# Counting the tokens above fifteen search steps: 24 matmuls of one tile each, or 3 matmuls of eight tiles each and a second matmul

## The reference

```python
cap = N // E                       # 3072 // 8 = 384
logits = x @ w_gate
order = np.argsort(-logits.flatten())
for idx in order:                  # best (token, expert) pairs first
    tok, e = (int(idx) // E, int(idx) % E)
    if assigned[tok] >= 0 or counts[e] >= cap:
        continue
    assigned[tok] = e
    counts[e] += 1
for e in range(E):
    mask = assigned == e
    out[mask] = np.maximum(x[mask] @ w1[e], 0.0) @ w2[e]
```

## Time and profile before

| | |
|---|---|
| time, median of 3 runs | 931.36 us (923.73 to 933.32) |
| profiled execution | 922.0 us, span 920.0 us |
| TensorE busy | 755.5 us, 82% of the span |
| TensorE weight loads | 563.7 us, 61% |
| VectorE busy | 464.4 us, 50% |
| ScalarE, GpSimd busy | 316.7 us, 221.6 us |
| chain that ended last | PE 63%, DVE 19%, issue 5%, DMA 4% |

### The profile page before, as it was taken

How to read it: one execution, slowest core, us unless ns; L and a number is a source line. 1 busy time by engine, 2 the same in 40 slices (tenths; PEclk the granted TensorE clock), 3 DMA queues, 4 the chain that set the end, 5 groups by cost and what they waited for, 6 DMA issues and landing times.

```text
span 920.0 us, 15204 instructions
## 1 busy us (share of the span) xinstructions
PE 755.5 (82%) x5546; PEld 563.7 (61%) x5546; DVE 464.4 (50%) x1172; ACT 316.7 (34%) x586; POOL 221.6 (24%) x281
## 2 busy tenths in 40 slices
PE   0077897998893169999999999999972999999994
PEld 0066887887783135565666565566542787777783
DVE  5989999999944737474747373632111000000010
ACT  9678787886610001111112121221210222222221
POOL 0455564645250010202020201223422000000000
PEclk9998979799896559999999999999995999999997
DMA  7293866768350303131414140641119999999970
GB/s 271 44 277 92 255 149 215 174 207 233 94 126 26 138 27 138 52 137 44 146 44 146 43 147 27 226 143 42 49 43 326 327 324 330 313 326 326 324 242 10
DMA packets 94040, 151.94 MB, mean 165 GB/s; under 512 B 21845, under 2 KB 71121, under 8 KB 93216
## 3 DMA queue, kind: packets, MB, share of 16 engines
q1 hardware_dynamic: 65728, 117.48, 38.3%
q0 software_dynamic: 11520, 24.03, 9.1%
q10 hardware_dynamic: 16736, 9.68, 3.6%
HBM read 115.92 MB, written 19.53 MB: 147 GB/s over the span
## 4 chain that ended last, share of the span: by engine, by line
PE 63%; DVE 19%; issue 5%; DMA 4%; ACT 3%; SPq 2%; POOL 1%; ACTq 1%; DVEq 0%; POOLq 0%
PE bank L867 15%; PE bank L880 14%; PE bank L996 10%; PE bank L1006 9%; PE bank L820 4%; PE bank L754 3%; DMA arena<-sorted 2%; DVE arena L1055 2%; SPq L245 2%; DVE arena L1095 2%; PE bank L904 2%; DVE arena L1070 1%; DVE arena L1142 1%; PE bank L856 1%; DVE arena L1126 1%
## 5 line engine op out<-in xcount | busy, mean ns | idle before, releaser
L867 PE MATMUL bank<-arena 128*128 128x384 f32 x384 | 140.3, 506 | 4.1 <-issue 3.4
L880 PE MATMUL bank<-arena 128*128 128x384 f32 x384 | 143.0, 503 | 0.0
L754 PE MATMUL bank<-arena 96*128 96x224 f32 (+1 forms) x384 | 92.7, 406 | 23.8 <-ACT arena L529 11.1
L996 PEld LDWEIGHTS bank<-arena 128*128 128x128 f32 x864 | 100.8, 194 | 5.5 <-issue 1.0
L996 PE MATMUL bank<-arena 128*128 128x128 f32 x864 | 101.0, 278 | 0.6 <-ACT arena L707 0.6
L754 PEld LDWEIGHTS bank<-arena 96*128 96x128 f32 x384 | 81.6, 231 | 29.7 <-issue 26.3
L1006 PE MATMUL bank<-arena 128*128 128x384 f32 x288 | 98.9, 486 | 0.0
L867 PEld LDWEIGHTS bank<-arena 128*128 128x128 f32 x384 | 68.8, 192 | 41.6 <-issue 6.0
L880 PEld LDWEIGHTS bank<-arena 128*128 128x128 f32 x384 | 67.3, 190 | 32.3
L344 POOL DMA_DIRECT2D arena<-arena x132 | 73.3, 566 | 53.8 <-DVE arena L1095 45.6
L408 POOL DMA_INDIRECT arena<-rows,arena x24 | 24.7, 1031 | 234.7 <-DVE arena L1303 229.5
(11 more groups left out here) (235 smaller groups left out, 1166.2 us busy)
## 6 DMA issues: line engine op xcount, KB each, us to landing
arena<-in_moe_w SPq DMA_DIRECT2D x52, 1536.0 KB, 7.7
arena<-arena POOLq DMA_DIRECT2D x48, 144.0 KB, 3.5
arena<-arena SPq DMA_DIRECT2D x46, 144.0 KB, 3.8
arena<-in_v SPq DMA_DIRECT2D x6, 1024.0 KB, 9.9
arena<-in_a_re SPq DMA_DIRECT2D x12, 384.0 KB, 4.2
arena<-in_a_im SPq DMA_DIRECT2D x12, 384.0 KB, 4.5
arena<-in_q SPq DMA_DIRECT2D x12, 384.0 KB, 6.7
arena<-in_k SPq DMA_DIRECT2D x12, 384.0 KB, 7.6
```

The lines of the kernel that those rows point to most:

```text
L754: mm = pe.matmul(bank[i][:, to:to + width], keys[p][0:SD, j * KW + e * P:j * KW + (e + 1) * P], queries[p][0:SD, from_:from_ + width], sta ...
L867: mm = pe.matmul(pP[f % 2][:, 0:CAP], w1_sb[p][:, kt * FF + f * P:kt * FF + (f + 1) * P], xeT[p][:, kt * CAP:(kt + 1) * CAP], start=(kt == ...
L880: mm = pe.matmul((pY, pKV)[m % 2][:, 0:DM], hT[p][:, f * CAP + t * P:f * CAP + (t + 1) * P], w2_sb[p][:, f * DM:(f + 1) * DM], start=(f == ...
L996: mm = pe.matmul(slot_hidden[f % 4][:, 0:width], w1_sb[p][:, kt * FF + f * P:kt * FF + (f + 1) * P], xeT[p][:, kt * width:(kt + 1) * width ...
```

## The change

For the 45 rounds that have other work between their steps, steps 2 to 5 of the round are replaced; the 11 others stay as they are. `count_grouped` takes eight token tiles in one matmul (`GT` = 8): 120 weight columns (8 tiles x 15 steps) against 64 columns (8 tiles x 8 experts), three matmuls instead of 24. The 120 x 64 result holds wanted blocks, where the tile of the row is the tile of the column, and unwanted ones. VectorE multiplies by a mask of the wanted ones (`own_tile`), sums over the tiles to 120 x 8, and spreads each row's sums to the 15 x 8 places of its step (`own_step`, 120 x 120). `add_groups` is one f32 matmul with weights of ones (120 x 128) on 120 columns, which gives every partition the whole 15 x 8 table. VectorE then takes the maximum over the experts, compares with 384, multiplies by the bound of the step, and the maximum of the reached bounds and the old prefix is the new prefix.

```diff
+        GT = P // (TH + 1)
+        GR = GT * TH
...
+        grouped_at = tied_tiles_at + NT * E
+
+        def handing_out(ph, d):
+            return ph >= 2 or ph == 1 and d >= 3
...
+            own = own_tile[:, :].rearrange("p (j e) -> p j e", e=E)
+            link(pool.memset(own_tile[:, :], 1.0))
+            link(pool.affine_select(out=own, in_=own, compare_op=ALU.is_ge, fill=0.0,
+                                    base=0, pattern=[[-TH, GT], [0, E]], channel_multiplier=1))
+            link(pool.affine_select(out=own, in_=own, compare_op=ALU.is_ge, fill=0.0,
+                                    base=TH - 1, pattern=[[TH, GT], [0, E]], channel_multiplier=-1))
+            link(pool.memset(own_step[:, :], 0.0))
+            for j in range(GT):
+                link(pool.affine_select(out=own_step[:, :], in_=own_step[:, :], compare_op=ALU.not_equal, fill=1.0,
+                                        base=-TH * j, pattern=[[-1, TH]], channel_multiplier=1))
+            link(pool.memset(ones_f[:, :], 1.0))
...
+            def count_grouped(r):
+                pe.wait_ge(ev("compared"), r + 1)
+                for g in range(NT // GT):
+                    mm = pe.matmul(search_bank[0:GR, grouped_at:grouped_at + GT * E], cmp_[:, g * GR:(g + 1) * GR],
+                                   co[:, g * GT * E:(g + 1) * GT * E], start=(g == 0), stop=(g == NT // GT - 1))
+                mm.then_inc(ev("counted"), 1)
+
+            def add_groups(r):
+                pe.wait_ge(ev("stepped"), r + 1)
+                pe.matmul(search_bank[:, totals_at:totals_at + TH * E], ones_f[0:GR, :], by_step[0:GR, :], start=True, stop=True)\
+                  .then_inc(ev("added"), 1)
...
+            plain = grouped = 0
             for ph in range(PHASES):
                 for d in range(DIGITS):
-                    busy = ph >= 2 or ph == 1 and d >= 3
-                    count(ph * DIGITS + d)
+                    busy = handing_out(ph, d)
                     if busy:
+                        count_grouped(ph * DIGITS + d)
                         fill(1)
-                    digit(ph * DIGITS + d)
-                    if busy:
+                        add_groups(grouped)
+                        grouped += 1
                         fill({3: 3, DIGITS - 1: 5}.get(d, 2))
+                    else:
+                        count(ph * DIGITS + d)
+                        digit(plain)
+                        plain += 1
...
+                link(dve.tensor_scalar(bounds, digits[:, dn * TH:(dn + 1) * TH], pre[cur], None, ALU.add))
+                link(dve.tensor_copy(reached[:, TH:TH + 1], pre[cur]))
+                dve.wait_ge(ev("counted"), rounds)
+                link(dve.tensor_tensor(own_part[0:GR, :], search_bank[0:GR, grouped_at:grouped_at + GT * E],
+                                       own_tile[0:GR, :], ALU.mult))
+                link(dve.tensor_reduce(own_counts[0:GR, :], tiles.rearrange("p j e -> p e j"), axis=AX.X, op=ALU.add))
+                dve.tensor_tensor(steps, own_step[0:GR, :].unsqueeze(2).broadcast_to([GR, TH, E]),
+                                  own_counts[0:GR, :].unsqueeze(1).broadcast_to([GR, TH, E]), ALU.mult)\
+                   .then_inc(ev("stepped"), 1)
+                if ph >= 1 and rounds - ph * DIGITS == 1:
+                    place_step(ph - 1, 6)
+                dve.wait_ge(ev("added"), grouped)
+                link(dve.tensor_reduce(most, search_bank[:, totals_at:totals_at + TH * E].rearrange("p (t e) -> p t e", e=E),
+                                       axis=AX.X, op=ALU.max))
+                link(dve.scalar_tensor_tensor(reached[:, 0:TH], most, float(CAP), bounds, ALU.is_ge, ALU.mult))
+                link(dve.tensor_reduce(pre[1 - cur], reached, axis=AX.X, op=ALU.max))
```

More of the change, by code:

```diff
@@ L109, in build @@
         padrow = sb("padrow", [P, RW], F32)
+        GT = P // (TH + 1)
+        GR = GT * TH
+        own_tile = sb("own_tile", [P, GT * E], F32)
+        own_step = sb("own_step", [P, TH], F32)
+        ones_f = sb("ones_f", [P, P], F32)
         g2_sb = sb("g2_sb", [P, KT * E2], F32)
@@ L169, in build @@
         flag = at(2, BF16)
+        own_counts, by_step = at(E), at(TH * E)
+        own_part, most, reached, bounds = at(GT * E), at(TH), at(TH + 1), at(TH)
         closed, full, open_, held, nte, ende, padf = (at(E) for _ in range(7))
@@ L1252, in _ @@
             link(dve.memset(made_rows[:, :, DM:RW], 0.0))
-            rounds = 0
+            rounds = plain = grouped = 0
             search_bank, place_bank = pT[1], pJ
@@ L1309, in name_expert, with steps_reached @@
                 dve.tensor_scalar(expert_no[:, n:n + 1], hp, -1.0, float(E), ALU.mult, ALU.add).then_inc(ev("expert_closed"), 1)
+            def steps_reached(cur, dn):
+                nonlocal grouped
+                grouped += 1
+                tiles = own_part[0:GR, :].rearrange("p (j e) -> p j e", e=E)
+                steps = by_step[0:GR, :].rearrange("p (t e) -> p t e", e=E)
+                link(dve.tensor_scalar(bounds, digits[:, dn * TH:(dn + 1) * TH], pre[cur], None, ALU.add))
[14 more added lines that the diff above has]
+                link(dve.tensor_reduce(pre[1 - cur], reached, axis=AX.X, op=ALU.max))
             def search(key, steps):
-                nonlocal rounds
+                nonlocal rounds, plain
                 cur = 0
@@ L1318, in search @@
                     dn = (4096, 256, 16, 1).index(step)
+                    busy = handing_out(ph, rounds - ph * DIGITS)
                     dve.scalar_tensor_tensor(cmp_.rearrange("p (n t) -> p n t", t=TH),
@@ L1323, in search @@
                     rounds += 1
+                    if busy:
+                        steps_reached(cur, dn)
+                        cur = 1 - cur
+                        continue
+                    plain += 1
                     dve.wait_ge(ev("counted"), rounds)
@@ L1328, in search @@
                         place_step(ph - 1, 6)
-                    dve.wait_ge(ev("digit"), rounds)
+                    dve.wait_ge(ev("digit"), plain)
                     link(dve.scalar_tensor_tensor(pre[1 - cur], search_bank[:, digit_at:digit_at + 1], float(step), pre[cur], ALU.mult, ALU.add))
```

## The result

| | before | changed |
|---|---|---|
| median of 4 runs | 927.55 us (921.41 to 933.32) | 939.02 us (935.6 to 940.34) |
| ratio | | 1.014 (95% interval 1.009 to 1.019) |
| measured again, one chip (11 and 6 runs) | 925.65 us | 937.34 us, ratio 1.0139 (1.011 to 1.017) |
| profiled execution: time, span | 922.0, 920.0 us | 935.6, 933.7 us |
| TensorE busy | 755.5 us, 82% | 737.0 us, 79% |

The change made the kernel slower, by 11.5 us in the medians and by 13.7 us in the two profiled spans. TensorE does 18 us less, and waits more than that.

What follows compares the result with a forecast made beforehand. TensorE was taken to bound the changed rounds before, the search's chain after. Terms summing to +5.4 us gave 927.4 for the profiled execution; added to the three-run median of 931.4 they gave 937 us, range 922 to 952.

Steps and rivals of the forecast that it cites:

- within 1%: Whole kernel: time within about 1% (9.3 us) of the kernel before, told as the same; chance 0.52.
- The bound moves from TensorE to the chain: Busy rounds: TensorE's 3.12 us falls to 2.35 to 2.5, and the search's chain of 3.11 us sets the pace.
- The chain, 3.11 us a round: New round, from one comparison's end to the next: the links through TensorE and VectorE sum to 3.11 us.
- Rounds 0 to 6 of five phases, +1.9 - 1.0: Phases 2 to 6: longer chain and `place_step` cost +1.9 us; TensorE's own stalls partly falling into new gaps give -1.0.
- 7 x 3.11: Rounds 0 to 6 of a phase: seven chain lengths, 21.8 us, set against the 21.51 us phase 3 took before.
- Round 7 and `count_found`, +2.7: Last round of a phase and what follows: count to total 5.27 us in phase 3; +0.45 x 6 = +2.7 us.
- Phase 1, +0.6 and 0.45: Phase 1: f32 matmul instead of the digit in rounds 3 and 4, +0.6 us; 0.45 us for its last round.
- The tables: nothing: GpSimd's 13 table instructions: at most 4 us, ready 14 us before VectorE wants them, so 0.
- The clock, +1.2: TensorE's clock: one more dip of 3.4 us at about half speed expected, +1.2 us.
- The clock rival: Busy rounds: the clock falls often, 4.7 us a round at 1.2 GHz; every second round hit gives +29, 966 us; chance 0.1.
- The slow-load rival: Grouped count: loads of 120 columns take 0.10 us each, not 0.03; chain 3.31, +8.6, in sum +14, 945 us; chance 0.3.
- The faster rival: Busy rounds: TensorE's relief counts, with a chain and rounds of 2.5 us; about 914 us; chance 0.1.

Runs made afterwards that it cites:

- the two runs with a link more: One VectorE copy of 128 x 24 added in the 45 busy rounds: to the kernel before, 926.01 us; to the changed kernel, 948.53 us.
- Two of the slower variants: The changed kernel with an added VectorE copy of 128 x 24 in 45 rounds, 948.53 us; the changed kernel with refine done twice, 947.53 us.

## Why the prediction was right or wrong

The time, 939.0 us, lies near 937 and in the range. The single most likely case was "within 1%", and the ratio, 1.014 (1.009 to 1.019), is most probably over that: the forecast's mechanism held, its size was too small. The two profiled executions differ by 13.7 us of span where the sum said 5.4; that the time came out so near is partly luck, since the difference was added to a median of three runs, 931.4, which lies above the 927.6 of four.

**The bound moves from TensorE to the chain: right**, by the two runs with a link more. TensorE's side was right too: the count 0.14 to 0.19 us (0.1 foreseen), `add_groups` 0.32 with its load (0.25, in which 0.04 for the load stood on no row). With three units at 0.67 that is 2.5 us of work in a round of 3.26, the share of 0.77 that was named as a sign. Of the other signs, the wait ahead of `add_groups` (0.49), rounds with transposes as long as the others and `count_found` waiting for VectorE came; VectorE still waits over 0.5 us in a round (0.57 for L855), which the prediction had ruled out.

**The chain, 3.11 us a round: measured 3.25 to 3.26.** VectorE's six instructions came as priced: 0.225, 0.267, 0.282, 0.283, 0.175, 0.170 us for 0.225, 0.27, 0.285, 0.28, 0.17, 0.165. The misses are both latencies of TensorE: count's start to VectorE 0.46 for 0.36, of which 0.09 is the slow load of 120 columns (0.37 with 128), and `add_groups` to VectorE 0.53 for 0.44. The second was priced from transposes that follow one another, with other work ahead of them; whether it is longer because TensorE has stood still before it was not tested.

**Rounds 0 to 6 of five phases, +1.9 - 1.0: measured +9.9.** From the first count of a phase to its last, in us:

| phase | 2 | 3 | 4 | 5 | 6 | sum |
|---|---|---|---|---|---|---|
| before | 22.33 | 21.51 | 21.29 | 21.96 | 22.97 | 110.1 |
| changed | 23.85 | 24.30 | 23.86 | 24.15 | 23.82 | 120.0 |

The step that failed is "7 x 3.11". Between rounds 3 and 4 stands `refine` with the reset of the prefix, five VectorE instructions of 1.08 us with links, and the sum left it out of the new rounds while it stood in the 21.51 us of phase 3 with which they were compared. Five phases times 1.08 are 5.4 us, and the two runs with refine twice show that the gap is open. The latencies make 0.14 us in each of 35 rounds, 4.9. With these the forecast's 5 x 21.9 = 109.5 comes to 119.8 of 120.0 measured. On the other side phase 3 was shorter than most: the five took 110.1, not 5 x 21.51 = 107.6. These 2.5 us, one dip of the clock among them, are what the -1.0 for stalls stood for. In sum 1.9 + 10.5 - 2.5 = 9.9.

**Round 7 and `count_found`, +2.7: measured +3.5** in phases 2 to 6, from the last count to L865 (`count_found`), less 0.1 a phase in what follows. Last count to total is 5.42 us in four of five phases, for 5.27. In phase 4 it is 5.77, in both executions of the changed kernel: VectorE began L1360 0.81 us after the count instead of 0.46, and nothing in the traces says why. With 128 weight columns, or with refine twice, that round has no such wait, but another round has (0.72 and 0.81 us).

**Phase 1, +0.6 and 0.45: measured +0.2** for all of it, by the first count of phase 2 (372.73 for 372.53 us).

**The tables: nothing, right.** The first count starts as before (286.44 for 286.41 us) and the plain rounds are unchanged.

**The clock, +1.2: measured -1, inside the +9.9.** There is one dip in each kernel within the busy phases, at 568 us before and at 431 us now, both to a granted clock of 0.53 for 3.4 to 3.6 us. A round took 4.26 us in the first (2.75 with the link more, without a dip), and 4.87 in the second (4.34 in the other phases). The waits in each round did not bring the clock down: over phases 2 to 6 it is 0.99 of 2.4 GHz. The clock rival is out. Two of the slower variants had three dips; whether their longer waits bring them is not shown.

**The slow-load rival** was half of the truth. Its load is real, 0.133 us against 0.098, but the matmuls of the group start 0.066 us apart, not 0.10, and it costs 0.09 a round and 4 us, not 0.2 and 8.6. Without it the kernel is still 1.0115 of before.

**The faster rival**: no link was more than 0.01 us under its price, and no busy round of phases 2 to 6 under 3.2 us.

## What to carry to other kernels

Where two engines answer each other round by round, price the chain through both, link by link, before taking work off the busy one: here TensorE's work in a round fell from 3.1 to 2.5 us, and the chain, 2.24 us and hidden before, became 3.26 us and set the pace. When a per-round price is multiplied, list what stands between the rounds on each engine as well; what is hidden there in the old kernel may be open in the new one, and what is in the old total must be in the new. And look at what a group costs beyond its own instructions: two groups of matmuls with small weights among full ones cost 0.39 us a round in this kernel, and full-size weights with unused columns and zero rows took that away without a new step in the chain (0.07 us a round more where TensorE had nothing else to do).

## What the runs showed of the hardware

- bf16 weight loads of 128 x 120 were recorded at 0.133 us and of 128 x 128 at 0.098; three matmuls of 64 columns started 0.066 us apart with the first and 0.034 with the second. Here more columns were faster.
- Between full-size matmuls a small-weight group costs about 0.1 us ahead of it and up to 0.1 behind it (unit before the digit 0.85 against 0.73, two units before the count 1.49 against 1.37; count 0.68 against 0.60, digit 0.10 against 0.03). The first load of the group started 0.17 and 0.33 us ahead of its matmul with full-size weights, and at the same time as it with weights of 15 rows or 15 columns.
- 24 matmuls of 8 columns took the same time from the first to the last with 15 and with 128 weight columns at a granted clock of 1.00 (0.585 and 0.580 us), and 0.587 and 0.641 at 0.50.
- A difference of 0.35 us in one wait of the changed kernel (phase 4, last round) has no cause that its traces show.
